# Summing value's first half fourth in the first two units of seven products, and turning the second half of the last output one position later

## What is computed

```python
def _attn_ref(q, k, v, tau):                      # q, k, v: 1 x 6016 x 256
    qn = q / (np.linalg.norm(q, axis=1, keepdims=True) + 1e-06)
    kn = k / (np.linalg.norm(k, axis=1, keepdims=True) + 1e-06)
    s = kn.transpose(0, 2, 1) @ qn / tau
    s = s - s.max(-1, keepdims=True)
    a = np.exp(s)
    a /= a.sum(-1, keepdims=True) + 1e-09
    return (v @ a).astype(np.float32)

def _moe_ref(x, w_gate, w_val, w_out, rms_g):     # 256 -> 1536 -> 256
    rms = np.sqrt(np.mean(x * x, axis=-1, keepdims=True) + 1e-06)
    xn = x / rms * rms_g
    g = xn @ w_gate
    silu = g * (1.0 / (1.0 + np.exp(-g)))
    val = xn @ w_val
    return (silu * val @ w_out).astype(np.float32)

def _moe2_ref(x, w_in, w_out):                    # 256 -> 2048 -> 256
    h = x @ w_in
    g = h - np.tanh(h)
    return (g @ w_out).astype(np.float32)
```

## Time and profile before

| | |
|---|---|
| time, median of 3 runs | 1172.57 us (1172.12 to 1173.0) |
| profiled execution | 1172.82 us, of it the span of the instructions 1170.7 us |
| PE | busy 1164.2 us, 99% |
| DVE | 909.5 us, 78% |
| ACT | 569.1 us, 49% |
| POOL | 173.5 us, 15% |
| DMA, mean over the span | 90 GB/s |
| block of weights (1024 KB), x60 | median 5.4 us from issue to landing |
| rows of the result (64 KB), x88 | median 1.8 us from issue to landing |

### The profile page before, as it was taken

One profiled execution on the slowest core, in us unless ns is written; L12 is line 12 of the kernel. 1 busy time (PEld: TensorE's weight loads), 2 busy tenths in 40 slices (PEclk: granted clock), 3 DMA queues, 4 the chain that ended last, 5 costly groups with the idle time before them and its releaser, 6 DMA issues.

```text
span 1170.7 us, 18228 instructions
## 1 busy us (share of the span) xinstructions
PE 1164.2 (99%) x5858; PEld 993.4 (85%) x5858; DVE 909.5 (78%) x1720; ACT 569.1 (49%) x835; POOL 173.5 (15%) x128
## 2 busy tenths in 40 slices
PE   9999999999999999999999999999999999999999
PEld 8888888888888888888888888888888888888998
DVE  6888697976977787787697697778778769769676
ACT  7866523365345435436435534544543643553442
POOL 4710000021012003003002101200300300210110
PEclk9999999999999999999999999999999999999999
DMA  9613555043025006106104302500600520430300
GB/s 368 216 59 105 149 121 180 1 140 113 1 89 163 0 14 201 36 0 179 72 0 141 110 0 90 161 0 16 199 36 0 175 72 0 126 108 1 118 10 14
DMA packets 132789, 104.82 MB, mean 90 GB/s; under 512 B 90640, under 2 KB 112784, under 8 KB 132752
## 3 DMA queue, kind: packets, MB, share of 16 engines
q1 hardware_dynamic: 132320, 103.83, 28.5%
q10 hardware_dynamic: 432, 0.52, 0.1%
HBM read 91.88 MB, written 12.45 MB: 89 GB/s over the span
## 4 chain that ended last, share of the span: by engine, by line
issue 71%; PE 17%; POOL 10%; DMA 1%; DVE 1%; SPq 0%; ACT 0%; POOLq 0%; DVEq 0%; ACTq 0%
POOL act L716 5%; PE ring L1508 5%; POOL act L719 5%; PE y_acc L1566 2%; PE out_acc L1566 2%; PE y_acc L1427 2%; PE ring L1559 2%; PE y_acc L1437 1%; PE out_acc L1622 1%; DMA qk_in<-in_q_dram 1%; DMA landing<-combined 1%; PE ring L1524 0%; PE y_acc L1628 0%; PE out_acc L1630 0%; SPq L532 0%
## 5 line engine op out<-in xcount | busy, mean ns | idle before, releaser
L827 ACT ACTIVATE act<-ring 128x512 f32<-128x512 f32 (+1 forms) x273 | 160.7, 589 | 300.0 <-PE ring L1508 271.8
L1508 PE MATMUL ring<-y_hi,wl 128*128 128x512 f32 (+1 forms) x712 | 241.2, 385 | 0.0
L1566 PE MATMUL out_acc<-h_hi,wl 128*128 128x512 f32 x704 | 239.8, 389 | 0.0
L1266 DVE TENSOR_TENSOR h_lo<-act,h_hi 128x512 fp32r<-128x512 f32 (+1 forms) x336 | 223.4, 677 | 7.1
L716 POOL TENSOR_TENSOR act<-gate_pair,act 128x512 f32<-128x512 f32 (+1 forms) x50 | 69.7, 1394 | 916.7 <-ACT act L876 916.7
L1176 DVE TENSOR_TENSOR act<-ring,act 128x512 f32<-128x512 f32 (+1 forms) x192 | 128.7, 671 | 56.7 <-ACT act L827 56.2
L1566 PEld LDWEIGHTS out_acc<-h_hi,wl 128*128 128x128 f32 x704 | 132.1, 188 | 27.6
L1508 PEld LDWEIGHTS ring<-y_hi,wl 128*128 128x128 f32 x712 | 133.4, 188 | 25.7
L1508 PE MATMUL ring<-y_lo,wl 128*128 128x512 f32 (+1 forms) x356 | 137.0, 385 | 0.0
L1566 PE MATMUL out_acc<-h_lo,wl 128*128 128x512 f32 x352 | 136.9, 389 | 0.0
L1566 PE MATMUL y_acc<-h_hi,wl 128*128 128x512 f32 (+1 forms) x384 | 126.4, 385 | 0.0
(11 more groups left out here) (232 smaller groups left out, 2036.6 us busy)
## 6 DMA issues: line engine op xcount, KB each, us to landing
landing<-combined SPq DMA_DIRECT2D x60, 1024.0 KB, 5.4
out_dram<-out_rows SPq DMA_DIRECT2D x88, 64.0 KB, 1.8
qk_in<-in_k_dram SPq DMA_DIRECT2D x9, 512.0 KB, 8.9
qk_in<-in_q_dram SPq DMA_DIRECT2D x9, 512.0 KB, 9.7
v_in<-in_v_dram SPq DMA_DIRECT2D x72, 64.0 KB, 2.4
w_in<-in_moe_w_out_dram SPq DMA_DIRECT2D x12, 256.0 KB, 2.9
combined<-wl SPq DMA_DIRECT2D x12, 256.0 KB, 4.2
combined<-w_in SPq DMA_DIRECT2D x12, 256.0 KB, 3.1
```

Of the source, the lines that this page charges most:

```text
L827: nc.scalar.activation(act[:, u % RING, 0:width], bank(t, name)[:, 0:width], func).then_inc(act_ready, 1)
L1266: nc.vector.tensor_tensor(h_lo[:, u % RING, 0:width], act[:, u % RING, 0:width], f32(h_hi[:, u % RING, 0:width]), ALU.subtract).then_inc(h ...
L1508: ins = nc.tensor.matmul(bank(t, name)[:, 0:width], weights(c, w_part), (hi if part else lo)[:, c, 0:width], start=c == 0 and w_part and part,
L1566: ins = nc.tensor.matmul(acc[:, d, 0:width], weights, (h_hi if part else h_lo)[:, u % RING, 0:width], start=f == 0 and w_part and part, st ...
```

## The change

Three things change, all in the tiles with seven products.

1. In units 0 and 2, DVE does value0 += its product fourth, behind gate1 = sum1 + u2, and value1, gate0 and gate1 follow as fifth, sixth and seventh. `SUMS_END` says after which step a half is finished, and all waits follow it: the value product of the odd unit behind waits for step 4 instead of 7; what waits for value1 waits for step 5 instead of 4, what waits for gate1 for step 7 instead of 6. From unit 4 on nothing changes. The order of PE, ACT, POOL and SP stays as it was, and value0's product stays PE's seventh.
2. POOL and DVE, in the second multiplication, wait for all seven steps (the same count as before).
3. `TURN_AT` says behind which unit a half of the last output is turned: in the two plain tiles behind units 0 and 1 as before, in tiles with seven products behind units 0 and 2.

```diff
--- before.py
+++ after.py
@@ -34,6 +34,8 @@
 FOLDED = 12
 WARM_START, WARM_COLUMNS = 12, 256
 V_TURN_AT, V_SPLIT_AT = 4, 7
+
+TURN_AT = ((0, 2), (0, 1))
 
 SEVEN_FROM = 2
 SEVENS = 6
@@ -489,7 +491,11 @@
 
         LAST_SEVEN = 2 * SEVENS - 2
 
-        BY_U2, BY_U3, BY_U4, BY_VALUE1, BY_GATE0, BY_GATE1, BY_VALUE0 = range(1, 8)
+        BY_U2, BY_U3, BY_U4 = 1, 2, 3
+        SUMS_END = ({"value1": 4, "gate0": 5, "gate1": 6, "value0": 7}, {"value0": 4, "value1": 5, "gate0": 6, "gate1": 7})
+
+        def ended(p, name):
+            return SUMS_END[p < LAG][name]
 
         def last_bank(t, p, name):
 
@@ -501,14 +507,14 @@
 
         LAST_OVER = ({"gate0": "sum1", "gate1": "sum2", "value0": "sum3"}, {"value0": "sum2"})
 
-        FIRST_LEFT = {"sum2": BY_U2, "sum1": BY_U4, "sum3": BY_VALUE1}
-        LAST_LEFT = {"gate0": BY_GATE0, "gate1": BY_GATE1, "value0": BY_VALUE0}
+        def first_left(p, name):
+            return {"sum2": BY_U2, "sum1": BY_U4, "sum3": ended(p, "value1")}[name]
 
         def steps_left(p, name):
             for last, over in LAST_OVER[p < LAG].items():
                 if over == name:
-                    return LAST_LEFT[last]
-            return FIRST_LEFT[name]
+                    return ended(p, last)
+            return first_left(p, name)
 
         def store_rows(eng, b, made, count):
 
@@ -715,7 +721,7 @@
                 pool.wait_ge(act_ready, t * U + p + 1)
                 nc.gpsimd.tensor_tensor(buf, gate_pair[:, 0:width], buf, ALU.mult).then_inc(seven_gated, 1)
                 pool.wait_ge(seven_gated, sevens(t, p, 1, 1))
-                pool.wait_ge(seven_step, sevens(t, p, STEPS, BY_VALUE0))
+                pool.wait_ge(seven_step, sevens(t, p, STEPS, STEPS))
                 nc.gpsimd.tensor_tensor(buf, value_pair[:, 0:width], buf, ALU.mult).then_inc(seven_made, 1)
 
             for t in range(SEVEN_FROM, TILES):
@@ -871,7 +877,7 @@
                     mark_seven(t, p // 2 + 1)
                 elif not last:
                     mark_seven(t + 1, 0)
-                act_e.wait_ge(seven_step, sevens(t, p, STEPS, BY_GATE1))
+                act_e.wait_ge(seven_step, sevens(t, p, STEPS, ended(p, "gate1")))
                 act_e.wait_ge(h_ready, t * U + (p - RING + 1))
                 nc.scalar.activation(act[:, p % RING, 0:width], gate_pair[:, 0:width],
                                      ACT.Sigmoid).then_inc(act_ready, 1)
@@ -1200,6 +1206,13 @@
                 dve.wait_ge(seven_full, sevens(t, p, PRODUCTS, SUM1))
                 nc.vector.tensor_tensor(gate1, of("sum1"), u2, ALU.add).then_inc(seven_step, 1)
                 dve.wait_ge(seven_step, sevens(t, p, STEPS, BY_U4))
+                def end_value0():
+                    dve.wait_ge(seven_full, sevens(t, p, PRODUCTS, VALUE0))
+                    nc.vector.tensor_tensor(value0, last_of("value0"), value0, ALU.add).then_inc(seven_step, 1)
+
+                if p < LAG:
+
+                    end_value0()
                 nc.vector.tensor_tensor(value1, of("sum3"), gate1, ALU.add).then_inc(seven_step, 1)
                 if p >= LAG:
 
@@ -1208,8 +1221,8 @@
                 nc.vector.tensor_tensor(gate0, last_of("gate0"), gate0, ALU.add).then_inc(seven_step, 1)
                 dve.wait_ge(seven_full, sevens(t, p, PRODUCTS, GATE1))
                 nc.vector.tensor_tensor(gate1, last_of("gate1"), gate1, ALU.add).then_inc(seven_step, 1)
-                dve.wait_ge(seven_full, sevens(t, p, PRODUCTS, VALUE0))
-                nc.vector.tensor_tensor(value0, last_of("value0"), value0, ALU.add).then_inc(seven_step, 1)
+                if p >= LAG:
+                    end_value0()
                 if p < LAG:
                     low()
 
@@ -1218,7 +1231,7 @@
                 dve.wait_ge(act_ready, t * U + p + 1)
                 nc.vector.tensor_tensor(buf, gate_pair[:, 0:width], buf, ALU.mult).then_inc(seven_gated, 1)
                 dve.wait_ge(seven_gated, sevens(t, p, 1, 1))
-                dve.wait_ge(seven_step, sevens(t, p, STEPS, BY_VALUE0))
+                dve.wait_ge(seven_step, sevens(t, p, STEPS, STEPS))
                 nc.vector.tensor_tensor(buf, value_pair[:, 0:width], buf, ALU.mult).then_inc(seven_made, 1)
 
             def sum_t(t, width, ns):
@@ -1363,8 +1376,8 @@
                     low_unit(t, u, width)
 
                 def beside(f):
-                    if f < KC:
-                        turn_out(t - 1, TILE, f)
+                    if f in TURN_AT[is_plain(t)]:
+                        turn_out(t - 1, TILE, TURN_AT[is_plain(t)].index(f))
                     if f == V_TURN_AT and not last:
                         turn_v(t + 1, ahead)
                     if f == V_SPLIT_AT - (0 if is_plain(t) else 1) and not last:
@@ -1543,12 +1556,12 @@
                         if not last:
                             free_bank(t, (name, p))
                         elif name in LAST_OVER[p < LAG]:
-                            pe.wait_ge(seven_step, sevens(t, p, STEPS, FIRST_LEFT[LAST_OVER[p < LAG][name]]))
+                            pe.wait_ge(seven_step, sevens(t, p, STEPS, first_left(p, LAST_OVER[p < LAG][name])))
                         elif p == 0:
 
                             pe.wait_ge(y_ready, t * KC)
                         else:
-                            pe.wait_ge(seven_step, sevens(t, p - 2, STEPS, BY_GATE1))
+                            pe.wait_ge(seven_step, sevens(t, p - 2, STEPS, ended(p - 2, "gate1")))
                         to = last_bank(t, p, name) if last else bank(t, (name, p))
                         for w_part, part in PASSES:
                             if isinstance(moves, tuple):
@@ -1674,7 +1687,7 @@
                                 pe.wait_ge(y_ready, t * KC)
                                 if not is_plain(t):
 
-                                    pe.wait_ge(seven_step, sevens(t, LAG - 1, STEPS, BY_GATE1))
+                                    pe.wait_ge(seven_step, sevens(t, LAG - 1, STEPS, ended(LAG - 1, "gate1")))
                         down("down", late, late, G, y_acc, y_full)
                     if is_seven(t, f):
                         seven_products(f, LAST_THREE, True)
```

## The result

The changed kernel takes 1214.6 us (median of four runs, 1212.47 to 1219.05) against 1172.34 us before: a ratio of 1.0365 (95% interval 1.0335 to 1.0394), 42.3 us slower. The forecast was 1204.6 us with a range of 1197 to 1212; the direction and the place are right, the size is 10 us short, and the time lies outside the range. The profiled execution took 1212.47 us, with a span of 1210.4.

The account below looks back on a forecast made before the run. PE, busy for 99% of the span, bounds the kernel, so new waits on it count. Nine full tiles at 3.05 us (27.5 us) plus 4.5 us in the last make 32.0 us: 1172.57 + 32.0 = 1204.6 us, range 1197 to 1212.

Parts of the forecast that it names:

- What bounds the kernel; the most that the sums can win: PE is busy for 99% of the span; removing value3's wait for value0 wins at most 6 us, 0.5%.
- The sums of units 0 and 2: On DVE and PE, the wait moves from value3 to sum1 of unit 2: +0.2 us a tile.
- The turning, 5.1 us later: On DVE, the second half is turned 5.1 us later than before, bounds 4.6 and 5.6.
- Load 3 and the chain behind it: Load 3, issued late on SP, delays ACT's rounding and PE's unit 6: 3.35 us in the example tile, 3.05 in full tiles.
- The last tile, 4.5 us: ACT and PE already wait for the load there, so the turning's whole delay, 4.5 us, passes through.
- Behind that, units 6 to 10 keep the old spacing at the later time: After the new wait in unit 6, PE's later units shift unchanged; loads 4 and 5 have room and PE cannot catch up.
- Faster (a): Late load 3 is covered and only value3's wait goes: 1166.6 us; chance 0.04.
- The same (b): Load 3 is covered and the wait moves from value3 to sum1: 1174.4 us; chance 0.03.
- Worse (c): Overlapping loads slow load 3 by 1 us, or the turning comes 1 us later, in each tile: 1214.6 us; chance 0.05.
- The Trainium skill's price of a DMA: 2.0 us plus bytes over 436 GB/s; load 3 would land 1.2 us sooner, the change cost about 12 us less; unused.

Follow-up runs that it names:

- the run with unit 2 alone: Kernel before the change with value0 summed fourth in unit 2 only, unit 0 and the turning as before: 1167.78 us, ratio 0.996.

## Why the prediction was right and where it fell short

*What bounds the kernel; the most that the sums can win.* Right. Value3's wait was worth 0.53 us a tile, and taking it away without a cost gave 4.9 us in the run with unit 2 alone.

*The sums of units 0 and 2.* Right, the net a little high. The product behind sum1 of unit 2 starts at 7.51 us of the tile, forecast 7.6; value3 no longer waits; the net is at most +0.06 us a tile in the first eight, forecast +0.2. The run with the sums alone shows the exchange: 1172.89 us.

*The turning, 5.1 us later.* Right: 5.0. It starts at 11.32 us of the tile, and the load behind it is issued at 14.26 instead of the forecast 14.3.

*Load 3 and the chain behind it.* Right in place, a little high: of the three tiles that kept their clock two are 2.7 us and one 2.95 us longer, forecast 3.05. The load took 5.5 to 5.7 us there against my mean of 5.6. The chain from the rounding's start to the product in question took 760.71 - 755.66 = 5.05 us, where I had put 5.15 together; ACT's two sigmoids follow each other in 0.54 us here, and I had taken 0.6.

*The last tile, 4.5 us.* Measured 4.84 us at unit 8, and it is that near by luck. Not the whole delay of the turning passed through: it began 4.4 us later (9.61 us into the tile instead of 5.19), load 3 was issued 3.7 us later (12.34 instead of 8.64) and ACT's rounding began 3.5 us later (18.17 instead of 14.63). The other 1.3 us came behind that, with a fall of the clock that the forecast did not have.

*"Behind that, units 6 to 10 keep the old spacing at the later time."* **This step failed.** I had put the new time of a tile together from durations at full clock and had taken PE's standstill as lost time and nothing else. In seven of ten tiles the products behind it ran at 1.2 GHz for a while. What a fall costs shows in two tiles whose loads took nearly the same time: own of unit 8 starts 31.35 us into the tile at 735.91 and 32.64 into the one at 535.77, where the rounding began 0.06 us later, so 1.2 us; the tile at 634.74, with a load 1.3 us longer and twice the time at the lower level, comes to 34.86. The run with idle matmuls puts the whole at 9.2 us of the 42.3, and gives 1205.4 us: the forecast of 1204.6 us was in effect that of the kernel with its clock held. The profile before had no such place to show: granted clock 1.000 in the mean, and in the last tile, the one with a wait of PE behind a load, it stood for only 0.41 us. I had no rival and no part of the range for it, though in all ten tiles the forecast put about 3 us of new standstill into less than 5 us of PE's time, between 640.4 and 645.17 in the example tile. The Trainium skill ("TensorE: Matmul & The Clock Gate", HAM oscillation) describes such a case, a matmul kernel whose PE waits for a load in each round and starts the next one throttled; by that case a fall belonged among the rivals, and the trace agrees in kind, with 0.50 granted from 658.5 to 665.2 us. It does not agree in size: the waits of that case are 3 to 5 us each, and in the changed kernel no single one was over 2.89 us.

*Rivals.* Faster (a) needed 3 us more room than there is. The same (b) is what the kernel does when SP's order is mended: 1172.65 us, forecast 1174.4. Worse (c) named 1214.6 us, the measured time, but for another reason, and is not confirmed by it: load 3 took 5.3 to 5.8 us in nine of the ten tiles, with load 5 issued only 2.5 us behind it, and 6.7 in one.

*The Trainium skill's price of a DMA* ("DMA: Bandwidth & Descriptors", Anatomy of one DMA), 4.4 us for 1 MB by its fit for GpSimd's transfers, was too low here: 5.46 us in the tile at 735.91, and 12 us less for the whole would have been further off.

## What to carry to other kernels

A step that ends in a DMA has two readers, its data's and the queue's: before moving it, read what stands behind its wait on the issuing engine. Here one order on SP made the late turning cost 29 us by itself and 42 us together with the new order of the sums; with the load put ahead of that wait, the late turning by itself gains 0.4%. And where a change puts a new standstill of a microsecond or more on a PE that was busy throughout, a fall of its clock behind it belongs in the range, at its own price.

## What was unexpected in the hardware

A PE that had been at full clock for 95 us was granted half of it from 658.5 us on, after it had stood for 2.17 us and worked for 0.7. In the last tile it fell behind 2.89 us, in the wait of 0.48 us that followed. In the other five with a fall no single wait was over 1.1 us; it came behind the first two, of at most 1.10 and 0.78 us, in one of the tiles behind a third of 0.11 us as well, though in the tile at 833.59, with 1.18, 0.78 and 0.19 us, it did not come. The same sequence, with waits of 0.92, 0.78 and 0.19 us in the tile at 735.91, left it at 1.00. So the length of the standstill does not tell by itself whether a fall comes (0.53, 0.75 and 0.11 us in the tile at 1030.56 had one), and the runs of one kernel scatter with it: 1212.47 to 1219.05 us for the changed kernel, 1172.33 to 1172.83 us for the one with load 3 ahead of the wait. Idle matmuls in the gaps took 9.2 us off the changed kernel and brought its scatter down to 0.5 us.
